# Sorting the first tokens of a scan-and-mixture kernel in two parts, and grouping the fp32 work of TensorE

## The chip, the cores and the metric

The kernel runs on one core of a Trainium2 chip. The metric is the device time of one execution in microseconds (us). Three runs of the kernel before gave 1382.56, 1383.54 and 1385.02 us (median 1383.54).

## What is computed

Three stages follow one another on N = 10112 tokens (2 sequences of 5056) of D = 256 values:

```
# stage A: a gated recurrence along each sequence
sig = 1.0 / (1.0 + np.exp(-f_logit))
f = lower_bound + (1.0 - lower_bound) * sig
h = f[:, t] * h + (1.0 - f[:, t]) * x[:, t]        # for t in range(S); y[:, t] = h
# layer 0: E = 8 experts of F = 1024, one expert for each token (cosine logits with tau)
xn = x / (np.linalg.norm(x, axis=-1, keepdims=True) + 1e-06)
logits = xn @ en.T / tau
expert_idx = np.argmax(logits, axis=1)
gate_w = softmax(logits)[arange(N), expert_idx]
out[mask] = gate_w[mask, None] * (np.maximum(x[mask] @ w1[e], 0.0) @ w2[e])   # per expert e
# layer 1: the same with other weights, and logits = x @ w_gate
```

## The kernel before

**Stage A, the scan.** Chunks of 512 tokens (CH = 4 tiles of P = 128; NCH = 20 chunks, the last of three tiles) are loaded as `xin` and `fin` (L737), transposed by TensorE (PE) into four PSUM banks (`a_front`, L1203: 16 transposes a chunk), and pass ScalarE's (ACT) tanh (L1049), GpSimd's (POOL) affine (L888) and VectorE's (DVE) product and scan (L371, L381). PE then transposes the result back (L1216) and computes the 8 logits of each token (L1222, `en_T`). ACT keeps the rows and their squares, and SP, the queue that issues most DMAs, stores the rows to `rows_a` in HBM (L745).

**A sort** puts the tokens of an expert together. A token's place ("slot") is found from counts: DVE finds the largest logit and a one-hot of the expert (`oh`, L413 to L419), PE counts with matmuls against ones and against an upper triangle (L1249, L1252), DVE turns the counts into slots (L432 to L464). Then a table "which row goes into which slot" is made. For each chunk of RC = 8 tiles, DVE and ACT build `tile_oh`, `lane_oh` and `vals` (`one_hots`, `scaled`), and PE accumulates 8 matmuls of 2 W columns (L1240). W is the number of 128-slot tiles that the table covers. Its two operands are read with a step of RC bf16 elements. DVE reads the table into `slot_row`. Each token's weight and number (`pair`) go to HBM as one store of 8 bytes a token beside the rows (`rows_a<-pair`, L813).

**The layers.** Slots are worked off in pairs of tiles (GW = 256 slots, one expert to a pair, NP = 47 pairs a layer, 94 in all). For each pair, SP reads the pair's expert from `expert` and loads 1 MB of `w1` and 1 MB of `w2` (`w1raw`, `w2raw`). ACT rounds them (`w1h`, `w2h`), and DVE takes the rest (`w1l`, `w2l`). POOL copies the pair's row numbers (`places`, L950) and gathers its rows by indirect DMA (`gather`, L966). PE transposes them (`turn_x`, L1290), and does `up` (L1306, 48 matmuls) and `down` (L1324, 48). In layer 0, ACT scales the result (`yb`), SP stores it to `rows_b`, and PE transposes it again (`turn_y`, L1344) and computes layer 1's logits (`y_logits`, L1335).

**What sets the order.** Each engine has its own written order. `step(i)` interleaves the work of pair i, of the pairs before it and of the next; each step has four points `tick(i, j)`, after the parts j = 0 to 3. A sort that runs beside the pairs is written as a generator on each engine, one `next` at each tick. Before, the first sort (`routing`, all TT = 79 tiles, W = 94) stands whole between scan and layer 0. The sort for layer 1 has two parts (`resort`): the first 64 tiles from step 34, for 16 whole pairs, and the rest from step 49, at the start of layer 1. Pair 0's weights are loaded at the end of the scan, as pair 0 always belongs to expert 0. POOL waits for `slot_row`, for the landing of the pair store and of the rows before it gathers.

Of the kernel before, what the change touches and what calls it, by code (L numbers as in the profile page):

```python
# [6 lines left out]
P = 128  # L7
# [45 lines left out]
def build(nc, x, f_logit, lower_bound, emb, tau, w1a, w2a, w_gate, w1b, w2b, out):  # L53
# [12 lines left out]
    G = 2  # L66
# [10 lines left out]
    UB = 2  # L77
    XA = 32
    GA = (N - (NP - XA) * GW - E * (GW - 1)) // GW
    TA, WA = G * XA, G * GA  # L80
# [12 lines left out]
    x_v = x.rearrange("b s d -> (b s) d").rearrange("(t p) d -> p t d", p=P)  # L93
    f_v = f_logit.rearrange("b s d -> (b s) d").rearrange("(t p) d -> p t d", p=P)

    ctx = ExitStack()
    with ctx:
# [7 lines left out]
        w1h = sb("w1h", [P, 2, WE], f32r)  # L105
        w1l = sb("w1l", [P, 2, WE], f32r)
        w2h = sb("w2h", [P, 2, WE], f32r)
        w2l = sb("w2l", [P, 2, WE], f32r)
# [25 lines left out]
        slot_tok = sb("slot_tok", [P, ST], fp32)  # L134
# [7 lines left out]
        hh = sb("hh", [P, JS, 512], f32r)  # L142
        hl = sb("hl", [P, JS, 512], f32r)
# [5 lines left out]
        sa = ExitStack()  # L149
        XS = UNROLL  # L150
        xin = sb("xin", [P, XS, CH * D], fp32, sa)
        fin = sb("fin", [P, XS, CH * D], fp32, sa)
        th = sb("th", [P, DC, CW], fp32, sa)
        fg = sb("fg", [P, DC, CW], fp32, sa)
        gx = sb("gx", [P, DC, CW], fp32, sa)
        sq = sb("sq", [P, 2, CH, D], bf16, sa)
        hT = sb("hT", [P, DC, 2, CW], fp32, sa)
        h_rows = sb("h_rows", [P, 2, CH * D], fp32, sa)
        sa.close()
# [3 lines left out]
        sr = ExitStack()  # L163
        lane_oh = sb("lane_oh", [P, RS, P, RC], bf16, sr)
        tile_oh = sb("tile_oh", [P, RS, ST, RC], bf16, sr)
        vals = sb("vals", [P, RS, 2 * ST, RC], bf16, sr)
        key = sb("key", [P, ST, E], fp32, sr)
        oh = sb("oh", [P, E, ST], bf16, sr)
        before = sb("before", [P, E, ST], fp32, sr)
        before2 = sb("before2", [P, E, ST], fp32, sr)  # L170
        small = sb("small", [P, 8, ST], fp32, sr)
        NORM_R, MAX_R, FIRST_R, SLOT_R, SUM_R, TMP_R, V0_R, OUT_R = range(8)
        ints = sb("ints", [P, 4, ST], i32, sr)
        e8 = sb("e8", [P, 8, E], fp32, sr)
        e8i = sb("e8i", [P, 2, E], i32, sr)
        cmp8 = sb("cmp8", [P, E, ST], fp32, sr)
        ex = sb("ex", [P, ST, E], fp32, sr)
        shifted = sb("shifted", [P, ST, E], fp32, sr)
        norm_e = sb("norm_e", [P, TT], fp32, sr)
        lane_rep = sb("lane_rep", [P, P, RC], bf16, sr)  # L180
        tile_rep = sb("tile_rep", [P, ST, RC], bf16, sr)
        where = sb("where", [P, 2, ST], bf16, sr)
        free = sb("free", [P, TA], bf16, sr)
        hole = sb("hole", [P, ST], fp32, sr)
        pair = sb("pair", [P, ST, 2], fp32, sr)
        sr.close()
# [3 lines left out]
        CUM_BANK, SUM_BANK = 2, 3  # L190
# [4 lines left out]
        pool_s = sem("pool_s")  # L195
        act_s = sem("act_s")
# [49 lines left out]
        PEEL_FIRST, PEEL_LAST = 3, 8  # L246
        SORT_FIRST, SORT_LAST = XA + 1, NP + GA - 2
# [3 lines left out]
        def part_of(r):  # L251

            if r == 0:
                return 0, TA, TA, WA, 0, GA
            return TA, ST, ST, ST - WA, GA, NP - GA

        def beside(part0, part1):

            def tick(i, j):
                if i.var is None and i.const * JS + j >= XA * JS + 2 * JS:  # L260
                    next(part0 if i.const < NP + 2 else part1, None)
            return tick

        FRONT = [18, 15]
# [26 lines left out]
        def run_pairs(eng, step):  # L291

            loop_layer[0] = 0
            run_steps(eng, 0, SORT_FIRST, step, PEEL_FIRST, 0, PAIR_UNROLL)
            loop_layer[0] = 1
            run_steps(eng, SORT_FIRST, LY * NP + 2, step, SORT_LAST - SORT_FIRST, PEEL_LAST, PAIR_UNROLL)
# [10 lines left out]
        CHUNK0 = [0, -(-TT // RC), -(-TT // RC) + -(-TA // RC), -(-TT // RC) + -(-TA // RC) + -(-ST // RC)]  # L307
# [3 lines left out]
        SPLIT_K = 3  # L311
        assert SPLIT_K + 1 < LOOP_K and NCH > LOOP_K + 4
# [5 lines left out]
        def _(dve):  # L318
# [32 lines left out]
            def split_w1_lo(i, c):  # L351

                cols = slice(c * F, (c + 1) * F)
                wait(dve, w1_hi, i.value(2, c + 1))
                v.tensor_tensor(w1l[:, par(i), cols], w1raw[:, par(i), cols],  # L355
                                w1h[:, par(i), cols].bitcast(fp32), ALU.subtract).then_inc(w1_lo, 1)

            def split_w2_lo(i, half):

                cols = slice(half * (WE // 2), (half + 1) * (WE // 2))  # L360
                wait(dve, w2_hi, i.value(2, half + 1))
                v.tensor_tensor(w2l[:, par(i), cols], w2raw[:, par(i), cols],  # L362
                                w2h[:, par(i), cols].bitcast(fp32), ALU.subtract).then_inc(w2_lo, 1)
# [31 lines left out]
            run_steps(dve, 0, edge_k, a_step, 6, 0)  # L395
            a_step(Index(edge_k), CH, edge_col)
            run_steps(dve, edge_k + 1, NCH - 1, a_step, max(LOOP_K - edge_k - 1, 0), 1)
# [1012 lines left out]
```

## Time and profile before

| | us |
|---|---|
| three runs, median | 1383.54 |
| the profiled execution, its own time | 1383.36 |
| its span, first to last instruction | 1381.6 |
| scan, to the last logits | 0 to 113 |
| first sort, to the first matmul of a pair | 113 to 169 |
| 94 pairs | 169 to 1380 |

PE is busy for 96% of the span, DVE 70%, ACT 60% and POOL 32%. Busy time says little of PE, whose matmuls overlap in the records. What counts is where PE waits, and how far the starts of its matmuls lie apart.

### The profile page before, as it was taken

The numbers are of one execution on the slowest core, as the hardware profiler recorded it, in microseconds if no ns is written. First come the engines' busy times: TensorE is split into PE (matmuls) and PEld (weight loads), VectorE is DVE, ScalarE is ACT, GpSimd is POOL, SyncE is SP. The second block draws the span as 40 slices with busy tenths as digits, with TensorE's granted clock in tenths as the row PEclk, the third lists the DMA queues.
The fourth block names the chain that finished last, engine by engine and source line by source line (L and its number), as shares of the span: only waits on it lengthen the run. The fifth ranks groups of instructions, "written<-read, shape, count | busy, mean of one in ns | idle before, by whom it ended". The sixth has DMA issues, their size and how long they took to land.

```text
span 1381.6 us, 31343 instructions
## 1 busy us (share of the span) xinstructions
PE 1329.6 (96%) x11005; PEld 1299.6 (94%) x11005; DVE 971.5 (70%) x1468; ACT 835.2 (60%) x1402; POOL 439.2 (32%) x458
## 2 busy tenths in 40 slices
PE   7994799999999999999999999999999999999996
PEld 6993399999999999999999999899999999999996
DVE  5878476666666666669876679777777777777773
ACT  4774166666666666666656566556666666666663
POOL 4663221121221211222111234323444444444431
PEclk9995599999999999999999999999999999999999
DMA  8983686666665656668856668546666666666650
GB/s 256 329 275 104 64 273 193 213 199 194 203 198 200 199 195 214 198 193 154 254 166 192 209 202 217 174 153 212 221 217 213 226 226 216 221 213 219 222 186 1
DMA packets 204662, 276.83 MB, mean 200 GB/s; under 512 B 33350, under 2 KB 171988, under 8 KB 204596
## 3 DMA queue, kind: packets, MB, share of 16 engines
q1 hardware_dynamic: 191060, 240.74, 56.7%
q0 software_dynamic: 13536, 35.21, 7.6%
q8 instruction: 41, 0.67, 0.2%
q14 instruction: 25, 0.20, 0.1%
HBM read 242.69 MB, written 35.18 MB: 201 GB/s over the span
## 4 chain that ended last, share of the span: by engine, by line
PE 91%; DVE 4%; issue 1%; ACT 1%; POOL 1%; DMA 1%; SPq 0%; ACTq 0%; DVEq 0%; POOLq 0%
PE bank L1306 39%; PE bank L1324 38%; PE bank L1240 4%; PE bank L1290 3%; PE bank L1335 2%; PE bank L1344 1%; PE bank L1203 1%; PE bank L1222 1%; PE bank L1216 1%; DVE hT L381 1%; DVE gx L371 1%; POOL fg L888 1%; ACT sq L1063 0%; DMA fin<-in_f_logit 0%; ACT th L1049 0%
## 5 line engine op out<-in xcount | busy, mean ns | idle before, releaser
L1306 PE MATMUL bank<-xs,w1h 128*128 128x256 f32 x3008 | 570.5, 288 | 1.5 <-DVE xs L656 1.5
L1119 ACT ACTIVATE hh<-bank 128x512 fp32r<-128x512 f32 x376 | 225.2, 599 | 413.6 <-PE bank L1306 413.6
L1306 PEld LDWEIGHTS bank<-xs,w1h 128*128 128x128 f32 x3008 | 461.5, 189 | 3.2 <-DVE xs L656 1.9
L667 DVE SCALAR_TENSOR_TENSOR hl<-bank,hh 128x512 fp32r<-128x512 f32 x376 | 259.9, 691 | 249.3 <-ACT hh L1119 246.9
L1324 PE MATMUL bank<-w2h,hl 128*128 128x256 f32 x1504 | 423.1, 281 | 0.0
L1324 PE MATMUL bank<-w2l,hh 128*128 128x256 f32 x1504 | 422.5, 281 | 0.0
L1324 PE MATMUL bank<-w2h,hh 128*128 128x256 f32 x1504 | 421.7, 280 | 0.0
L1306 PE MATMUL bank<-xs,w1l 128*128 128x256 f32 x1504 | 421.6, 280 | 0.0
L1306 PEld LDWEIGHTS bank<-xs,w1l 128*128 128x128 f32 x1504 | 283.7, 189 | 0.0
L1324 PEld LDWEIGHTS bank<-w2h,hh 128*128 128x128 f32 x1504 | 283.3, 188 | 0.0
L1324 PEld LDWEIGHTS bank<-w2l,hh 128*128 128x128 f32 x1504 | 283.1, 188 | 0.0
L1324 PEld LDWEIGHTS bank<-w2h,hl 128*128 128x128 f32 x1504 | 283.0, 188 | 0.0
L355 DVE TENSOR_TENSOR w1l<-w1raw,w1h 128x1024 fp32r<-128x1024 f32 x188 | 230.2, 1225 | 45.0 <-ACT w1h L1032 44.8
L362 DVE TENSOR_TENSOR w2l<-w2raw,w2h 128x1024 fp32r<-128x1024 f32 x188 | 230.4, 1226 | 43.1 <-ACT w2h L1040 42.2
L966 POOL DMA_INDIRECT xb<-rows_a,row_i x94 | 110.2, 1172 | 459.1 <-DVE meta L660 440.8
L976 POOL DMA_INDIRECT out_y<-yb,tok x94 | 125.8, 1338 | 313.0 <-DVE tok L675 282.9
L1032 ACT ACTIVATE w1h<-w1raw 128x1024 fp32r<-128x1024 f32 x188 | 197.6, 1052 | 7.1 <-DMA w1raw<-in_moe_w 7.1
L1040 ACT ACTIVATE w2h<-w2raw 128x1024 fp32r<-128x1024 f32 x188 | 197.6, 1052 | 0.8 <-DMA w2raw<-in_moe_w 0.8
L966 POOL DMA_INDIRECT xb<-rows_b,row_i x94 | 107.7, 1146 | 67.0 <-DVE meta L660 29.7
L1135 ACT ACTIVATE yb<-bank,meta 128x256 f32<-128x256 f32 x188 | 78.6, 470 | 11.4 <-PE bank L1324 4.5
L656 DVE TENSOR_TENSOR xs<-bank,xs 128x512 fp32r<-128x512 f32 x94 | 64.9, 690 | 11.5 <-ACT xs L1113 8.9
L1240 PE MATMUL bank<-vals,lane_oh 128*128 128x124 bf16 (+2 forms) x237 | 59.3, 415 | 10.7 <-DVE vals L511 10.5
(160 smaller groups left out, 1039.6 us busy)
## 6 DMA issues: line engine op xcount, KB each, us to landing
w1raw<-in_moe_w SPq DMA_DIRECT2D x94, 1024.0 KB
w2raw<-in_moe_w SPq DMA_DIRECT2D x94, 1024.0 KB, 5.6
rows_b<-yb SPq DMA_DIRECT2D x94, 128.0 KB, 2.3
xin<-in_x SPq DMA_DIRECT2D x19, 512.0 KB, 6.0
fin<-in_f_logit SPq DMA_DIRECT2D x19, 512.0 KB, 7.9
rows_a<-h_rows SPq DMA_DIRECT2D x19, 512.0 KB, 5.6
xb<-rows_a,row_i POOLq DMA_INDIRECT x94, 4.9
xb<-rows_b,row_i POOLq DMA_INDIRECT x94, 4.9
```

The lines of the kernel that those rows point to most:

```text
L355: v.tensor_tensor(w1l[:, par(i), cols], w1raw[:, par(i), cols], w1h[:, par(i), cols].bitcast(fp32), ALU.subtract).then_inc(w1_lo, 1)
L362: v.tensor_tensor(w2l[:, par(i), cols], w2raw[:, par(i), cols], w2h[:, par(i), cols].bitcast(fp32), ALU.subtract).then_inc(w2_lo, 1)
L667: v.scalar_tensor_tensor(hl[:, j, :], bank[j % UB][:, :], 0.0, hh[:, j, :].bitcast(fp32), ALU.max, ALU.subtract).then_inc(hid_lo, 1)
L966: pool.indirect_dma_start(xb[:, s, :], None, rows_of(i), bass.IndirectOffsetOnAxis(row_i[:, s:s + 1], 0)).then_inc(x_in[s], 16)
L976: pool.indirect_dma_start(out, bass.IndirectOffsetOnAxis(tok[:, s:s + 1], 0), yb[:, s, :], None, bounds_check=N - 1, oob_is_err=False).the ...
L1032: nc.scalar.activation(w1h[:, par(i), cols], w1raw[:, par(i), cols], ACT.Copy).then_inc(w1_hi, 1)
L1040: nc.scalar.activation(w2h[:, par(i), cols], w2raw[:, par(i), cols], ACT.Copy).then_inc(w2_hi, 1)
L1119: nc.scalar.activation(hh[:, j, :], bank[j % UB][:, :], ACT.Relu).then_inc(hid_hi, 1)
L1135: nc.scalar.activation(yb[:, s, :], bank[Y_BANK + par(i)][:, t * D:(t + 1) * D], ACT.Copy, scale=meta[:, bass.ds(in_layer(i).value(2 * G, ...
L1240: ins = mm(bank[b][:, 0:2 * W], lane_oh[:, g % RS, :, t], vals[:, g % RS, 0:2 * W, t], start=first and t == 0, stop=last and t == w - 1)
L1306: ins = mm(bank[j % UB][:, f * GW:(f + 1) * GW], w[:, p, o:o + P], xs[:, p, a, c * GW:(c + 1) * GW], start=k == 0, stop=k == 3 * DC - 1)
L1324: ins = mm(bank[Y_BANK + p][:, t * D:(t + 1) * D], a[:, j, f * GW + t * P:f * GW + (t + 1) * P], w[:, p, o:o + D], start=(j, t, f, k) == ( ...
```

## The change

1. The first sort has two parts. Part 0 takes the first K1 = 10 chunks (T1 = 40 tiles, 5120 tokens) and gives only whole pairs of one expert: P1 = 12 pairs, W = 24. It stands between scan and layer 0, where `routing` stood. Part 1 takes all 79 tiles for the other 35 pairs (W = 70); tokens already placed are masked. It runs at the ticks of steps 0 to 9 of layer 0, which are now written out instead of looped.
2. As pair 0's expert is no longer known beforehand, SP reads the experts of pairs 0 and 1 and loads both pairs' weights once part 0 has found the experts. The pair store of part 0 comes behind these four loads.
3. Both sorts of a layer are one generator (`sort(q)`, q = 0 to 3). Parts 1 and 3 count two experts at a time (four rounds between PE and DVE, in one bank), parts 0 and 2 four. Part 2 starts at step 35, part 3 at step 50.
4. In layer 0, `turn_y` (both tiles) and `y_logits` (both tiles, in a bank of their own, a step later) stand together behind `turn_x`. Before, they stood at four places of a step.
5. `xin` and `fin` are loaded so that a partition holds four consecutive tokens, 4 KB in one piece instead of four of 1 KB. The transposes put them back in order of time by writing every fourth column of the PSUM bank.
6. The number tables of POOL (`lane_rep`, `tile_rep`) are made ahead of the scan. `w1h` and the others are two buffers each, so that pair 0's lie apart from the scan's buffers.

```
-        SORT_FIRST, SORT_LAST = XA + 1, NP + GA - 2
+        PARTS = [(0, T1, T1, G * P1, 0, P1), (T1, TT, TT, ST - G * P1, P1, NP - P1),
+                 (0, TA, TA, G * PA, 0, PA), (TA, ST, ST, ST - G * PA, PA, NP - PA)]
+        FRONT = [20, 21, 22, 21]
+        OH_AT = [2, 2, 4, 2]
+        EXPERTS_AT_ONCE = [4, 2, 4, 2]
...
+            def tick(i):
+                if i.var is None and i.const >= NP + 3:
+                    next(parts[3], None)
+                elif i.var is None and i.const >= XA + 3:
+                    next(parts[2], None)
+                elif i.var is None and i.const < XA:
+                    next(parts[1], None)
...
 # SP
-                if i.var is None and i.const == NCH - 1:
-                    load_w1(Index(0))
-                    load_w2(Index(0))
+            def sort(q):
+                lo, hi = PARTS[q][0:2]
+                for _ in range(OH_AT[q] + 2 * len(groups(q)) + 6):
+                    yield
+                if q == 0:
+                    sp.wait_ge(dve_c, mark["experts", q])
+                    for i in (Index(0), Index(1)):
+                        read_expert(i)
+                        load_w1(i)
+                        load_w2(i)
+                        yield
+                sp.wait_ge(dve_c, mark["pair", q])
+                sp.dma_start((rows_av if q < 2 else rows_bv)[:, lo:hi, D:D + 2], pair[:, lo:hi, :]
+                             ).then_inc(pair_out, 16)
...
 # POOL, ahead of the first gather
-            pool.wait_ge(dve_c, mark["slots"])
+            pool.wait_ge(dve_c, mark["slots", 0])
             pool.wait_ge(pair_out, 16)
...
 # PE, a_front
+                        in_time = dst[:, 0:nt * P].rearrange("p (q j) -> p q j", j=nt)
                         for j in range(nt):
-                            ins = nc.tensor.transpose(dst[:, j * P:(j + 1) * P],
+                            ins = nc.tensor.transpose(in_time[:, :, j],
...
 # PE, the counting matmuls of a sort
+                for b, e, k, number in groups(q):
+                    if b == 0:
+                        pe.wait_ge(dve_c, mark["oh", q])
+                    else:
+                        pe.wait_ge(dve_c, mark["counted", q, b - 1])
+                    mm(sum_of(q, T), ones_b[:, :], oh[:, e:e + k, 0:T], start=True, stop=True)
+                    mm(cum_of(q, T), upto[:, :], oh[:, e:e + k, 0:T], start=True, stop=True).then_inc(pe_s, 1)
...
 # PE, step(i), behind turn_x
+                if here(old) and layer_of(old) == 0:
+                    y_logits(old)
                 if here(last2) and layer_of(last2) == 0:
-                    y_logits(last2, 1)
-                tick(i, 1)
+                    turn_y(last2)
+                tick(i)
```

SP's queue between the last stores of the scan (`rows_a<-h_rows`) and layer 0, before: pair 0's weights first, then the pair store, then pair 1's weights once the experts are read.

```order
L745 DMA rows_a<-h_rows 128x3x256 [waits rows_ok]
L759 DMA w1raw<-in_moe_w 128x2x1024
L767 DMA w2raw<-in_moe_w 128x8x256
L813 DMA rows_a<-pair 128x79x2 [waits dve_c]
L772 TENSOR_LOAD expert [waits dve_c]
```

The same place after:

```order
L719 DMA rows_a<-h_rows 128x3x256 [waits rows_ok]
L742 TENSOR_LOAD expert [waits dve_c]
L746 ISA
L729 DMA w1raw<-in_moe_w 128x2x1024
L746 ISA
L737 DMA w2raw<-in_moe_w 128x8x256
L742 TENSOR_LOAD expert
L746 ISA
L729 DMA w1raw<-in_moe_w 128x2x1024
L746 ISA
L737 DMA w2raw<-in_moe_w 128x8x256
L782 DMA rows_a<-pair 128x40x2 [waits dve_c]
```

No load stands ahead of the experts any more, and the pair store, of 40 tiles, has moved behind four loads of 1 MB.

PE in a step of layer 0 before, around `turn_x` (L1290), with one `y_logits` (L1335) behind it; the other `y_logits` and the two `turn_y` stand between other `up` and `down` groups.

```order
L1324 MATMUL bank<-w2l,hh 128x256
L1324 MATMUL bank<-w2h,hl 128x256
L1290 MATMUL bank<-ident,xb 128x128 x4
L1335 MATMUL bank<-wg_T,yT 128x8 x2
L1306 MATMUL bank<-xs,w1h 128x256 x2
L1306 MATMUL bank<-xs,w1l 128x256
```

The same place of a step in which part 1 of the first sort builds its table, after:

```order
L1269 MATMUL bank<-w2l,hh 128x256
L1269 MATMUL bank<-w2h,hl 128x256
L1235 MATMUL bank<-ident,xb 128x128 x4
L1282 MATMUL bank<-wg_T,yT 128x8 x4
L1292 MATMUL bank<-ident,yb 128x128 x4
L1214 MATMUL bank<-vals,lane_oh 128x140 x8
L1251 MATMUL bank<-xs,w1h 128x256 x2
L1251 MATMUL bank<-xs,w1l 128x256
```

All of a step's fp32 work is now one run, and behind it stand 8 table matmuls of 140 columns; there are ten such groups of up to 8 (79 matmuls) at the ticks of steps 5 to 8.

## Rows read from the trace of the kernel before

**Rows 1.** Windows by stage; the first row names the columns.
```profile
core 0: us, PE busy (x) PEld busy (x) DVE busy (x) ACT busy (x) POOL busy (x), PEclk, DMA share, GB/s
109.00:169.00 60.00, 33.20 (x105) 16.07 (x105) 41.34 (x82) 16.34 (x24) 16.54 (x12) 0.50 0.48 64
303.00:316.00 13.00, 13.00 (x114) 13.00 (x112) 8.42 (x13) 8.11 (x14) 2.43 (x3) 1.00 0.60 202
832.00:845.00 13.00, 12.70 (x107) 12.24 (x106) 12.06 (x21) 7.46 (x12) 5.64 (x5) 1.00 0.64 213
```

**Rows 2.** The chain in order of time, scan to layer 0: start, us, what.
```profile
116.38 3.10 DVE oh L419
...
123.03 0.18 DVE e8i L440
...
131.31 26.90 PE bank L1240 x79
...
158.52 0.27 DVE slot_row L485
...
163.71 3.11 DMA xb<-rows_a,row_i
...
169.04 5.02 PE bank L1306 x24
```

**Rows 3.** The chain in order of time, one step of layer 0.
```profile
303.19 0.44 PE bank L1290 x4
303.62 0.35 PE bank L1335 x4
303.97 1.51 PE bank L1306 x12
...
306.90 0.22 PE bank L1344 x2
307.12 1.40 PE bank L1306 x12
```

**Rows 4.** Timeline of DVE in the sort of 64 tiles beside layer 0.
```profile
615.71 0.68 DVE L535 TENSOR_REDUCE small<-logit 128x64 f32<-128x512 f32 x1
...
628.78 2.60 DVE L548 TENSOR_TENSOR oh<-key,small 128x512 bf16<-128x512 f32 x1
...
662.30 1.07 DVE L606 TENSOR_REDUCE small<-before 128x64 f32<-128x512 f32 x1
...
678.64 0.69 DVE L507 TENSOR_TENSOR lane_oh<-lane_rep,where 128x1024 bf16<-128x1024 bf16 x1
```

**Rows 5.** Timeline of SP: first and last of the four loads before layer 0.
```profile
165.96 0.39 SPq L759 DMA_DIRECT2D w1raw<-in_moe_w  x1
...
167.98 1.41 SPq L767 DMA_DIRECT2D w2raw<-in_moe_w  x1
```

**Rows 6.** DMA issues: KB each, median us to landing; third and fourth at 168 to 183.
```profile
rows_a<-pair SPq DMA_DIRECT2D x1, 79.0 KB, 15.3
rows_b<-pair SPq DMA_DIRECT2D x1, 64.0 KB, 14.8
...
w2raw<-in_moe_w SPq DMA_DIRECT2D x1, 1024.0 KB, 14.3
...
xb<-rows_a,row_i POOLq DMA_INDIRECT x5, 6.6
```

**Rows 7.** The chain, table matmuls beside layer 0 (64 columns) and layer 1 (124).
```profile
685.16 0.97 PE bank L1240 x8
...
908.90 1.84 PE bank L1240 x8
```

**Rows 8.** The chain in the scan: logits, and transposes at full and at half clock.
```profile
52.24 1.69 PE bank L1222 x16
...
68.57 1.80 PE bank L1203 x16
...
87.87 3.26 PE bank L1203 x16
```

More of the change, by code:

```diff
@@ L147, in build @@
         yT = sb("yT", [P, 2, D], fp32)
-        sa = ExitStack()
         XS = UNROLL
[L151 to L159, printed above, removed]
+        th = sb("th", [P, DC, CW], fp32)
@@ L161, in build @@
+        fg = sb("fg", [P, DC, CW], fp32)
+        gx = sb("gx", [P, DC, CW], fp32)
+        sq = sb("sq", [P, 2, CH, D], bf16)
         RC = 8
         RS = 4
[L163 to L169, printed above, removed]
@@ L180, in build @@
[L180 to L186, printed above, removed]
+        WM = ST - G * min(P1, PA)
+        lane_oh = sb("lane_oh", [P, RS, P, RC], bf16)
+        tile_oh = sb("tile_oh", [P, RS, WM, RC], bf16)
+        vals = sb("vals", [P, RS, 2 * WM, RC], bf16)
@@ new lines, in build @@
+        shifted = sb("shifted", [P, ST, E], fp32)
+        norm_e = sb("norm_e", [P, TT], fp32)
+        lane_rep = sb("lane_rep", [P, P, RC], bf16)
+        tile_rep = sb("tile_rep", [P, WM, RC], bf16)
+        where = sb("where", [P, 2, ST], bf16)
+        free = sb("free", [P, max(T1, TA)], bf16)
+        hole = sb("hole", [P, ST], fp32)
+        pair = sb("pair", [P, ST, 2], fp32)
+        scan_only = ExitStack()
+        xin = sb("xin", [P, XS, CH * D], fp32, scan_only)
+        fin = sb("fin", [P, XS, CH * D], fp32, scan_only)
@@ L1231, in _ @@
+            parts = [sort(q) for q in range(2 * LY)]
             run_steps(pe, 0, NCH, a_step, LOOP_K, 2)
             a_back(Index(NCH - 1), tiles_in(NCH - 1))
-            def chunk(g, w, W, b, first, last):
-                pe.wait_ge(lane_ok, g + 1)
-                pe.wait_ge(valp_ok, g + 1)
-                pe.wait_ge(valt_ok, g + 1)
-                for t in range(w):
-                    ins = mm(bank[b][:, 0:2 * W], lane_oh[:, g % RS, :, t], vals[:, g % RS, 0:2 * W, t],
-                             start=first and t == 0, stop=last and t == w - 1)
-                ins.then_inc(tab_ok, 1)
@@ L1358, in step @@
                     down(last, 2)
-                if here(last2) and layer_of(last2) == 0:
-                    turn_y(last2, 1)
-                tick(i, 0)
+                tick(i)
                 if here(i):
@@ L1373, in step @@
                     down(i, 0)
-                if here(last) and layer_of(last) == 0:
-                    turn_y(last, 0)
-                tick(i, 2)
+                tick(i)
                 if here(i):
```

664 lines of the change are left out of this document (308 added, 356 removed).

## The prediction

> **What bounds the kernel now.** I read the windows by stage first, then the chain that ended last. In layer 0 PE is busy for 13.00 of 13 us at full clock while DVE is busy for 8.42 [rows 1], and the chain of a step consists of PE groups that follow one another without a gap [rows 3]. So PE bounds both layers, and what DVE, ACT, POOL or a transfer does there costs nothing until it holds PE up. The windows give the margin too: where a sort runs beside the pairs, DVE is busy for 12.06 of 13 us [rows 1]. Between scan and layer 0 it is the other way round. PE is busy for 33.2 of 60 us at clock 0.50, the 1.2 GHz level [rows 1], and the chain goes through DVE's counting, 79 table matmuls (26.90), `slot_row`, the gather and the first `up` at 169.04 [rows 2]. The sort starts at S = 113.0, some 3.4 us ahead of `oh` at 116.38, so the lead-in is 56.0 us long. In the scan itself the chain goes through PE and the engines behind it, not through the loads: transposes 1.80 and logits 1.69 stand in it [rows 8].
>
> All changes are set against the profiled execution: span 1381.6, its own time 1383.36, 1.8 more; the median of the runs is 1383.54, 0.2 above that.
>
> **Start of the scan.** `xin` and `fin` in pieces of 4 KB land a little earlier, but only the first chunk is waited for: −0.3 (−0.6 to 0). The transposes into every fourth PSUM column I cost at nothing, and keep their price as a rival. POOL's number tables go where POOL was idle.
>
> **Lead-in, from S.** The first part sorts 40 tiles, 320 numbers a partition. DVE's wide operations shrink from 640 numbers: `oh` took 3.10 [rows 2], and 2.60 for 512 [rows 4], some 0.5 per 128 numbers, so 1.8. The lines of 512 numbers at 0.68 and 1.07 [rows 4] become about 0.5 and 0.7. Maximum to `oh` is then about 3.8, the norm 0.6, two counting rounds with PE 2.4, nine operations on 8 experts such as `e8i` at 0.18 [rows 2] 1.85, and the experts of the pairs 0.85: experts at S + 9.5. The slots take DVE another 9 or so, and five chunks of one-hots at 1.05 each (`lane_oh` 0.69 [rows 4] and a third of the other) 5.3. PE's 40 table matmuls of 48 columns hide behind these: 26.90/79 for 188 columns is 1.8 ns a column [rows 2], so 40 × 48 × 1.8 ns = 3.5. `slot_row` is ready at S + 24.2, against 45.5 before (158.52 [rows 2]).
>
> But POOL waits for the pair store too, and this is where the queue matters. SP issues four loads of 1 MB once the experts are there, then the pair store. Before, such four went from 165.96, the last issued at 167.98 and landed 14.3 later [rows 5, 6], so 16.3 from first to last, gathers among them; without gathers I take 14.5. The pair store is behind them in the queue. It took 15.3 for 79 tiles and 14.8 for 64 [rows 6]. In proportion to the tiles 40 would take 7.7, by the line through the two 14.0. The issue and the first descriptors pass beside the loads, so I take 6.5 behind them. That gives S + 9.5 + 14.5 + 6.5 = S + 30.5, 6 us after the slots: **the end of the pair store takes the place of the slots**. Then row numbers (0.9), two gathers beside what is left of the traffic at 6.6 (the median [rows 6]; 3.11 alone [rows 2]) and transposes, rounding and start of `up` 2.2: first `up` at S + 40.2. Against S + 56.0 that is −15.9. Bounds: −21.5, slots at S + 24.2 and nothing else late; −12, a store that takes nearer 14.
>
> **Part 1 on PE in layer 0.** Of the 79 table matmuls none is saved. They are 140 columns wide now and stand between PE groups that never wait. Eight took 0.97 at 64 columns and 1.84 at 124 [rows 7], 0.0145 a column; at 140 that is 1.84 + 16 × 0.0145 = 2.07. Then 79/8 × 2.07 = 20.4. The eight counting matmuls add 0.7 and a wait at the first chunk 0.3: +21.4, less 0.1 as the last group is one matmul short: +21.3 (20 to 24). This is the term that decides: what was beside nothing, 26.90 in the lead-in, costs 20 in a place where PE is full.
>
> **DVE in steps 0 to 3.** The key, `oh` and exp work of part 1 on 640 numbers is about 4.6 in one step, on top of 8.8 of split work: 13.3 against a step of 11 to 13 without `turn_y`. PE stalls +1.2 (0 to 4). Steps 6 and 7 have four chunks of one-hots each, for DVE some 4 × 1.1 on top of 8.42 [rows 1], in a step that four groups of table matmuls stretch to 21; that fits. The slots stand at the ticks of step 8 and POOL reads them at step 9, a step of some 13 us later: no wait.
>
> **fp32 work together.** Before, a step has `turn_x` 0.44, two logits matmuls 0.35 (four records, two to a matmul), and `up` behind them 1.51 where it is 1.40 elsewhere: 0.11 for going back. `turn_y` 0.22 stands apart, with `up` behind it at 1.40 [rows 3]. With the second logits and `turn_y` that comes to 0.44 + 2 × 0.35 + 2 × 0.11 + 2 × 0.22 = 1.80. After, the logits are eight records in a row. In the scan 16 in a row take 1.69 [rows 8], 0.106 each against 0.35/4 = 0.088, so eight take 0.80 to 0.85: 0.44 + 0.80 + 0.44 + 0.11 = 1.79. If two groups of 0.35 stay what they are, it is 1.69. The ends for 47 steps are thus −5 and, with 0.85, +2; I take −1.5. It is a small gain, since `turn_y` had no delay behind it to give up.
>
> **Second sort.** Part 3 counts in four rounds, a step apart, and starts a step later: −0.2 (−0.5 to +0.5), both within what DVE had free.
>
> **Sum.** −0.3 − 15.9 + 21.3 + 1.2 − 1.5 − 0.2 = +4.6. Span 1386.2, with 1.8 around it 1388.0, +0.3%.
>
> **Rivals.** *A, the pair store is not in the way.* Its descriptors might be carried beside the four loads, or the loads be so far down that it lands before the slots. The first `up` then comes by the slots: S + 24.2 + 0.9 + 3.1 to 6.6 + 2.2, near S + 34.5 with part of the contention. That is −21.5 instead of −15.9, in all 1382.4; with the −5 end of the fp32 work 1379. So it ends at not slower, or faster. For it: 79 tiles took 15.3 alone, 64 took 14.8 beside layer traffic, so traffic hardly slowed it [rows 6]. Against: that traffic was not four loads ahead in its own queue. It decides from where the store lands before S + 25, 15.5 us after the experts. 0.25.
>
> *B, the strided transposes are slow.* The transposes now write fp32 columns 16 bytes apart. No row shows such a write. If each took as long as at half clock, 3.26 in place of 1.80 for 16 [rows 8], the 20 chunks would cost 20 × 1.46 = 29 less what slack PE has in a chunk, some 0.2 to 0.4: +25, in all 1412. It decides from about 0.4 us a chunk, beyond PE's slack. Against it: a matmul's output is written once a column, 1.8 ns apart at most when strided operands are read [rows 7], and ACT and POOL read the bank packed as before. The Trainium skill, Advanced Engine Details and Errata, section PSUM Cachelines, says that any non-contiguous access pattern significantly slows down matmuls, with lines of two fp32 values; no run here has yet shown it. By that rule the time would be near this rival's, without it the forecast's. 0.11.
>
> *C, DVE or gathers too late in steps 0 to 5.* The pair store of 39 tiles in step 4 and DVE's 4.6 of extra work fall where weights for the next pairs must be split. Two or three steps that end on DVE at 13.3 to 15 instead of PE at 11 to 13 cost +5, in all 1392. The store of 64 tiles cost PE nothing beside layer 0, where PE stayed full. 0.07.
>
> *D, the change does not do what it says.* The slots of part 1 come too late for pair 12, so the pairs wait for the sort after all, for half a step or more: 1395. A step between writing and reading speaks against it. 0.03.
>
> **How the numbers follow.** The forecast has 0.54: 1388.0, by itself 1384 to 1393 from the ends of the lead-in (−21.5 to −12) and of DVE and fp32. A's times reach from 1379 to 1384. The range is 1380 to 1393: it leaves out B, D and the lowest part of A. A measurement of this kernel tells 0.2%, 2.8 us, from no change: faster is below 1380.8, slower above 1386.3. Faster takes half of A and little of the forecast, 0.14; within 0.2% the rest of A and a third of the forecast, 0.28; slower two thirds of the forecast with B, C and D, 0.58.
>
> **What would show it.** Lead-in: the gather's end in the chain comes from `pair_out` and not from `slot_row`; the pair store lands some 6 us after the slots; first `up` 40 us after S. If the chain goes through `slot_row`, A is right. Part 1: nine groups of table matmuls near 2.07 and one of 7 in the chain of steps 5 to 8; steps 6 and 7, with four each, near 21 us. DVE: an idle stretch of PE in step 0 or 1 that ends on `w1l`, `w2l` or `h`. fp32: in layer 0's chain `turn_x` 0.44, logits x8 0.80, `turn_y` 0.44 and `up` behind them 1.51; logits of 0.70 would show the end of −5. Scan: 1.80 a group of 16 transposes, with S still near 113; at 3 or above, B. I would be wrong at the root if table matmuls of 140 columns between `up` groups took nearer 1 us for eight, or if first `up` came later than S + 44.

## The result, and the profile after

The changed kernel took 1389.4 us (median of 6 runs, 1386.44 to 1395.21) against 1383.9 for the kernel before (6 runs): ratio 1.0045, 95% interval 1.0034 to 1.0057. In a later series of 10 runs it took 1386.6 against 1384.1: 1.0018, interval 1.0008 to 1.0028. So it is slower, by 0.2 to 0.5% (2.5 us in one series, 5.5 in the other); the forecast was 1388.0, +0.3%.

The profiled execution happened to be the slowest of the first series (1395.21, span 1393.5). The profile of the second series (1386.23, span 1384.5) is near the median and stands for the changed kernel from here on, called the second profile. The lines of code are numbered anew: `turn_x` is L1235, `up` L1251, `down` L1269, `y_logits` L1282, `turn_y` L1292, the table matmuls L1214, the counting matmuls L1201 and L1202.

The difference to the kernel before, stretch by stretch, from the starts of `turn_x` of single pairs in both traces (us):

| stretch | before | after, second profile | difference |
|---|---|---|---|
| start to `turn_x` of pair 0 | 165.30 | 152.41 | −12.9 |
| to pair 2 | 20.30 | 23.75 | +3.5 |
| pairs 2 to 6 | 51.95 | 50.31 | −1.6 |
| pairs 6 to 9 (tables of part 1) | 39.29 | 59.37 | +20.1 |
| pairs 9 to 34, plain steps of layer 0 | 327.32 | 323.95 | −3.4 |
| pairs 34 to 62 (second sort, change of layer) | 380.62 | 380.77 | +0.2 |
| pairs 62 to 92, plain steps of layer 1 | 353.60 | 350.90 | −2.7 |
| rest | 43.2 | 43.0 | −0.2 |

Chain of the second profile from scan to layer 0 (start, us, what), beside [rows 2]:

```profile
113.28 0.18 DVE logit L434
...
123.25 0.18 DVE expert L535
...
126.83 18.17 DMA rows_a<-pair
145.13 0.31 POOL row_i L912 x2
...
146.03 6.24 DMA xb<-rows_a,row_i
152.41 1.10 PE bank L1235 x4
```

S, the end of the copy of the last logits, is 113.5. The experts stand at S + 9.9, the pair store lands at S + 31.5, and the first `up` begins at 154.90, S + 41.4. The slots were ready long before: `slot_row` ends at 137.3, S + 23.8. Nothing of the table matmuls is in the chain; the store is.

One plain step of layer 0 in its chain, beside [rows 3], and table matmuls of 140 columns, beside [rows 7]:

```profile
389.68 0.44 PE bank L1235 x4
390.12 0.79 PE bank L1282 x8
390.91 0.49 PE bank L1292 x4
391.40 1.41 PE bank L1251 x12
...
255.24 2.07 PE bank L1214 x8
```

The windows of the second profile, beside [rows 1]: the lead-in is shorter and still at the 1.2 GHz level, the layer is as full as before.

```profile
core 0: us, PE busy (x) PEld busy (x) DVE busy (x) ACT busy (x) POOL busy (x), PEclk, DMA share, GB/s
108.00:155.00 47.00, 10.85 (x70) 8.77 (x70) 27.49 (x78) 10.34 (x27) 7.49 (x10) 0.51 0.66 166
385.00:398.00 13.00, 13.00 (x114) 13.00 (x113) 8.46 (x12) 8.11 (x12) 2.16 (x3) 1.00 0.61 205
```

What was open: how much of the result is noise of the scan, whether the store is really what the gather waits for, what the stall ahead of pair 2 is, why plain steps of **both** layers became shorter though only layer 0's fp32 work was moved, and whether the table matmuls must cost 20 us.

### The profile page after: what moved, and what is told of

Read it like the earlier page. It is cut to its first block, busy times and chain, and to the rows that moved or that the text cites. A ratio compares the mean times of both kernels' runs of the same rounds, so it can differ in the third digit from the quotient of the medians.

```text
span 1393.5 us, 31206 instructions
## 1 busy us (share of the span) xinstructions
PE 1326.5 (95%) x11057; PEld 1304.2 (94%) x11057; DVE 984.9 (71%) x1497; ACT 826.0 (59%) x1361; POOL 419.3 (30%) x461
## 4 chain that ended last, share of the span: by engine, by line
PE 91%; DVE 4%; DMA 2%; issue 1%; POOL 1%; ACT 1%; DVEq 0%; POOLq 0%; ACTq 0%
PE bank L1269 38%; PE bank L1251 38%; PE bank L1214 4%; PE bank L1235 3%; PE bank L1282 3%; PE bank L1164 2%; PE bank L1183 2%; PE bank L1292 2%; DMA rows_a<-pair 1%; PE bank L1177 1%; DVE hT L426 1%; DVE gx L416 1%; POOL fg L860 0%; DMA xb<-rows_a,row_i 0%; DVE oh L487 0%
## 5 line engine op out<-in xcount | busy, mean ns | idle before, releaser
L1251 PE MATMUL bank<-xs,w1h 128*128 128x256 f32 x3008 | 559.7, 285 | 1.4 <-DVE xs L618 1.4
L1251 PEld LDWEIGHTS bank<-xs,w1h 128*128 128x128 f32 x3008 | 464.6, 190 | 4.4 <-DVE xs L618 1.8
L1269 PE MATMUL bank<-w2h,hl 128*128 128x256 f32 x1504 | 422.4, 281 | 0.0
L1269 PE MATMUL bank<-w2h,hh 128*128 128x256 f32 x1504 | 421.9, 281 | 0.0
L1251 PE MATMUL bank<-xs,w1l 128*128 128x256 f32 x1504 | 421.8, 280 | 0.0
L1269 PE MATMUL bank<-w2l,hh 128*128 128x256 f32 x1504 | 421.6, 280 | 0.0
L1251 PEld LDWEIGHTS bank<-xs,w1l 128*128 128x128 f32 x1504 | 285.0, 189 | 0.0
L1269 PEld LDWEIGHTS bank<-w2h,hh 128*128 128x128 f32 x1504 | 283.9, 189 | 0.0
L1269 PEld LDWEIGHTS bank<-w2h,hl 128*128 128x128 f32 x1504 | 283.7, 189 | 0.0
L1269 PEld LDWEIGHTS bank<-w2l,hh 128*128 128x128 f32 x1504 | 283.7, 189 | 0.0
L928 POOL DMA_INDIRECT xb<-rows_a,row_i x94 | 96.5, 1027 | 488.3 <-DVE meta L622 457.7
L938 POOL DMA_INDIRECT out_y<-yb,tok x94 | 123.0, 1308 | 313.1 <-DVE tok L640 283.1
L928 POOL DMA_INDIRECT xb<-rows_b,row_i x94 | 101.3, 1078 | 69.5 <-DVE meta L622 42.2
L1235 PE MATMUL bank<-ident,xb 128*128 128x128 f32 x376 | 56.8, 274 | 16.9 <-DMA xb<-rows_a,row_i 16.9
```

The costliest lines, as they stand in the source:

```text
L928: pool.indirect_dma_start(xb[:, s, :], None, rows_of(i), bass.IndirectOffsetOnAxis(row_i[:, s:s + 1], 0)).then_inc(x_in[s], 16)
L938: pool.indirect_dma_start(out, bass.IndirectOffsetOnAxis(tok[:, s:s + 1], 0), yb[:, s, :], None, bounds_check=N - 1, oob_is_err=False).the ...
L1235: ins = nc.tensor.transpose(bank[X_BANK][:, o:o + P], xb[:, s, c * P:(c + 1) * P], ident[:, :])
L1251: ins = mm(bank[j % UB][:, f * GW:(f + 1) * GW], w[p][:, o:o + P], xs[:, p, a, c * GW:(c + 1) * GW], start=k == 0, stop=k == 3 * DC - 1)
L1269: ins = mm(bank[Y_BANK + p][:, t * D:(t + 1) * D], a[:, j, f * GW + t * P:f * GW + (t + 1) * P], w[p][:, o:o + D], start=(j, t, f, k) == ( ...
```

## The experiments

Ratios are to the kernel before, in the same series.

**The changed kernel again.**

> The changed kernel once more. Its profiled execution took 1395.21 us, 5.8 above its median 1389.4, and its scan ended 6.6 us later than that of the kernel before. Theory 1 (the late scan belongs to that execution, the changed loads cost little): here the last logits are kept within 2 us of 113, the profiled time is 1387 to 1391, and the steps of the layers are the same as before to 0.02 us. Theory 2 (the changed loads and transposes cost it): the scan ends at 117 or later again.

1386.59 us, ratio 1.0018 (1.0008 to 1.0028), 10 runs. The scan ends at 113.3, as theory 1 has it. In the first profile it ended at 119.4, and the chain shows where that came from:

```profile
20.60 3.21 PE bank L1183 x16
23.81 3.51 PE bank L1164 x16
```

In the second profile the same two groups stand at 20.35 with 1.69 and at 22.04 with 1.80. In every profile PE's first groups take twice the time of later ones (3.66 for 16 transposes at 8.44 before, 3.58 at 9.96 after), up to 19 or 20 us; in this one it goes on to 28. These are the durations that stretches at the half clock have in [rows 8], though the windows print a granted clock of 1.00 for that stretch. Of the nine profiles with the changed start four have it (the first, and those of the old loads, of the store first and of the changed kernel with the tables in rows); their last logits are copied at 117.0 to 119.4. The five others with that start (112.2 to 114.3) and the five with the start as before (110.2 to 112.8) don't. What differs at the start is one operation. DVE's `emb_q` took 0.40 us before and takes 2.66 now, since POOL makes `lane_rep` and `tile_rep` at that moment, from the chain and the timeline of POOL in the second profile:

```profile
6.43 2.66 DVE emb_q L383
...
5.94 1.94 POOL L879 IOTA lane_rep<- 128x1024 bf16 x1
7.83 1.10 POOL L879 IOTA tile_rep<- 128x560 bf16 x1
```

PE's first transposes begin at 9.96 instead of 8.44. That the later start makes the long slow stretch more frequent fits all 14 profiles, but four in nine against none in five can be chance, and it was not tried by itself.

The traces differ in one more place. In four of them (the first profile and, of the experiments below, the old loads, the store first and `vals` in rows) the granted clock falls to half once, for some 3 us, among the table matmuls of part 1. In the first three of these PE does not wait there, and pairs 6 to 9 take 60.8 to 60.9 us, against 59.4 in the second profile. Single executions of the changed kernel so differ by several us for reasons that the change does not fix, and the stretches of the table above are the surer ground.

**fp32 work apart again.**

```
 # PE, step(i), of the changed kernel; ACT and DVE follow
+                if here(last2) and layer_of(last2) == 0:
+                    turn_y(last2, 1)                      # behind down(last, 2)
...
-                if here(old) and layer_of(old) == 0:
-                    y_logits(old)
                 if here(last2) and layer_of(last2) == 0:
-                    turn_y(last2)
+                    y_logits(last2, 1)
```

> The changed kernel with the fp32 work of layer 0 at four places of a step, as before the change. A plain step of layer 0 took 13.09 us before and 12.96 after; one of layer 1, which has no such work, 11.79 and 11.70. Theory 1 (grouping gives 0.04 a step, the rest has another cause that acts in both layers): layer 0 steps of 13.00 to 13.01, layer 1 steps still 11.70, the kernel 2 us slower than the changed one. Theory 2 (grouping gives the whole 0.13): layer 0 steps of 13.09, 6 us slower.

1387.56 us, ratio 1.0028 (1.0014 to 1.0041). Pairs 9 to 34 take 325.60 us, 13.02 a step, against 323.95, 12.96. So grouping gives 0.066 a step, 3.1 us in 47 steps. The medians of the two kernels (1387.56 and 1386.59) are too close to show so much; it rests on the steps, which repeat to 0.01 us from trace to trace. The 0.066 is half of the 0.13 by which the steps of layer 0 became shorter. Steps of layer 1 are 11.70 in both. Theory 1 holds. In the chain of this kernel the delay behind logits is there again, and none behind `turn_y`:

```profile
404.23 0.35 PE bank L1281 x4
404.57 1.48 PE bank L1252 x12
...
407.48 0.22 PE bank L1290 x2
407.69 1.37 PE bank L1252 x12
```

**The weights placed as after.**

```
-        w1h = sb("w1h", [P, 2, WE], f32r)
+        w1h = [sb("w1h0", [P, WE], f32r)]
...
         pair = sb("pair", [P, ST, 2], fp32, sr)
+        for n, t in (("w1h", w1h), ("w1l", w1l), ("w2h", w2h), ("w2l", w2l)):
+            t.append(sb(n + "1", [P, WE], f32r, sr))
+        hh = sb("hh", [P, JS, 512], f32r, sr)
+        hl = sb("hl", [P, JS, 512], f32r, sr)
```

> The kernel before with one edit: the rounded weights are two buffers each, and the second ones and hh and hl stand at the end of SBUF, as after the change. Theory 1 (matmuls of up and down take 113 ns instead of 117 to 120 for some positions of their operands in SBUF): steps of layer 1 about 11.70 instead of 11.79, of layer 0 about 13.00 instead of 13.09, the kernel 6 to 8 us faster than before, near 1376. Theory 2 (the gain of 0.09 a step comes from the rewritten order of the steps): steps as before, time as before.

1388.56 us, ratio 1.0034 (1.0024 to 1.0044): slower. Steps of layer 0 take 13.16 instead of 13.09, of layer 1 11.81 instead of 11.79. Neither theory: places alone do move every step, but this placement, which is not the changed kernel's to the byte, moves them the other way. The next experiment on this is the last one.

**Loads and transposes of the scan as before.**

```
-                        in_time = dst[:, 0:nt * P].rearrange("p (q j) -> p q j", j=nt)
-                            ins = nc.tensor.transpose(in_time[:, :, j],
+                            ins = nc.tensor.transpose(dst[:, j * P:(j + 1) * P],
```

> The changed kernel with xin and fin loaded in pieces of 1 KB and transposes that write 128 columns in a row, as before the change. Theory 1 (both edits of the scan are about free): 16 transposes at full clock 1.80 us in either, end of the scan within 1 us of that of the changed kernel in the same clock, total within 2 us. Theory 2 (writes into every fourth PSUM column are slow, rival B of the prediction): the changed kernel would be slower than this one, by 5 us or more.

1389.8 us (6 runs), ratio 1.0038 (1.0021 to 1.0055), not faster than the changed kernel. At full clock 16 transposes take 1.80 us in this kernel, in the changed one and in [rows 8], and its profile has the long slow stretch at 20 to 28 us too (3.21 and 3.51). So neither the 4 KB pieces nor the writes into every fourth PSUM column have a price that can be seen, and they are not what makes the scan late. The Trainium skill, Advanced Engine Details and Errata, section PSUM Cachelines, has any non-contiguous access slow matmuls significantly; for fp32 transposes written 16 bytes apart the two traces do not show it.

**The pair store first.**

```
+                sp.wait_ge(dve_c, mark["pair", q])
+                sp.dma_start((rows_av if q < 2 else rows_bv)[:, lo:hi, D:D + 2], pair[:, lo:hi, :]
+                             ).then_inc(pair_out, 16)
                 if q == 0:
-                    sp.wait_ge(dve_c, mark["experts", q])
                     for i in (Index(0), Index(1)):
```

(The same two statements behind the loop are gone.)

> The changed kernel with the pair store of part 0 ahead of the four weight loads in SP's queue instead of behind them. In the second run of the changed kernel the slots were read at S + 24, the pair store landed at S + 31.7 and the first up began at S + 41.6. Theory 1 (the store waits behind the loads in its queue and holds the gather): it lands before the slots, the chain goes through slot_row, first up near S + 32 to S + 34, the kernel 8 to 9 us faster than the changed one, near 1379. Theory 2 (8-byte packets are slow wherever they stand, and weights are needed as much): the landing moves to S + 25 at best, the loads come 4.3 us later and the first up waits for w1l, gain under 4 us.

1382.43 us, ratio 0.9993 (0.9976 to 1.001). S is 117.5 in its profile, after the slow stretch. The store lands 9.8 us after its issue at 128.73, at S + 21.0, ahead of the slots (S + 23.8). The first `up` begins at 152.13, S + 34.6, and the gather now starts behind the slots:

```profile
139.98 0.93 PE bank L1213 x8
...
141.61 0.32 POOL row_i L911 x2
...
143.63 6.34 DMA xb<-rows_a,row_i
...
152.13 2.94 PE bank L1250 x12
```

That is 6.8 us earlier against S than in the changed kernel, and up to pair 2 nothing of it comes back (21.07 us from first `up` to the third `turn_x`, against 21.26). So the mechanism is theory 1. The gain in time, though, is not the 8 to 9 us expected: against the kernel before, the medians are 0.1 us lower here and 2.5 or 5.5 higher for the changed kernel, a gain of 2.6 to 5.6 with runs that spread from 1376.5 to 1387.4. The two variable stretches named above (slow start, clock among the tables) are both in this profile; how much of the shortfall they are in the other runs was not traced. The windows show why the place in the queue matters: in the second profile of the changed kernel the loads move 373 GB/s with the store behind them, and from 138 on it is alone, with a DMA share of 2.00 for 8 GB/s (the share adds up the times of packets, and can exceed 1). With the store first it has that phase at 130, while DVE still counts. Two rows of the changed kernel, then one of this one:

```profile
130.00:132.00 2.00, 0.00 (x0) 0.00 (x0) 1.83 (x9) 0.45 (x1) 0.00 (x0) 0.50 1.11 373
138.00:140.00 2.00, 0.00 (x0) 0.00 (x0) 2.00 (x3) 1.29 (x2) 0.00 (x0) 0.50 2.00 8
```

```profile
130.00:132.00 2.00, 0.00 (x0) 0.00 (x0) 1.90 (x8) 0.00 (x0) 0.00 (x0) 0.50 0.76 13
```

**Part 1 two ticks later.**

```
-        FRONT = [20, 21, 22, 21]
-        OH_AT = [2, 2, 4, 2]
+        FRONT = [20, 23, 22, 21]
+        OH_AT = [2, 4, 4, 2]
...
-                if q == 2:
+                if q in (1, 2):
                     yield
```

> The changed kernel with part 1 of the first sort two ticks later from its key on, so that PE's first counting matmul (which waited 4.5 us for DVE's oh at step 1, and 2.4 for the masked oh) stands two ticks, half a step, later. Theory 1 (PE's stall of steps 0 and 1 is that wait): from first up to the third turn_x 17 to 18.5 us instead of 21.3, the kernel 3 us faster than the changed one. Theory 2 (DVE is simply overloaded there, and another of its products would be waited for, w1l or hl): still 20 to 21 us, no change in time.

1382.85 us, ratio 1.0007 (0.9996 to 1.0018), 0.3 us above the kernel before where the changed kernel is 2.5 above: a gain of 2.2, 3 expected. The expectation named a wrong wait: the 4.5 us for `oh` belong to part 0, in the lead-in. Part 1's is the wait for the masked `oh` (L490). From first `up` to the third `turn_x` it takes 16.7 us instead of 21.3, so theory 1 holds. Of these 4.6 us only 2.4 were idle. The windows of the changed kernel and then of this one show the rest, PEclk is the third number from the end:

```profile
164.00:168.00 4.00, 2.38 (x21) 2.19 (x19) 3.97 (x6) 1.55 (x2) 1.82 (x1) 1.00 0.81 262
168.00:172.00 4.00, 3.20 (x22) 3.21 (x23) 3.61 (x7) 1.28 (x2) 1.88 (x3) 0.79 0.28 71
172.00:176.00 4.00, 4.00 (x29) 4.00 (x29) 2.39 (x5) 1.31 (x3) 0.00 (x0) 0.79 0.78 258
```

```profile
164.00:168.00 4.00, 4.00 (x36) 4.00 (x36) 3.96 (x7) 1.67 (x3) 2.52 (x2) 1.00 0.87 276
168.00:172.00 4.00, 4.00 (x37) 4.00 (x36) 3.96 (x5) 2.77 (x4) 1.40 (x2) 1.00 0.62 192
172.00:176.00 4.00, 3.78 (x34) 3.55 (x33) 3.86 (x9) 2.95 (x6) 0.73 (x1) 1.00 0.74 203
```

Behind the wait the granted clock is 0.79 for 8 us: part of them ran at 1.2 GHz again, right after the clock had come back. That does not follow each time. In the kernel with the fp32 work apart PE waits 2.3 us at the same place and in the one with `vals` in rows (below) 2.1, and in both the clock stays at full speed. From first `up` to the third `turn_x` they take 19.7 us, against 16.6 before and 21.3 here. One group behind the wait, in the second profile and in the kernel with the fp32 work apart:

```profile
168.80 0.24 PE bank L1201
...
170.68 2.56 PE bank L1269 x12
```

```profile
169.72 0.24 PE bank L1202
...
171.49 1.41 PE bank L1270 x12
```

So of the 4.6 us some 2.4 are the wait and 1.6 the clock. The last 0.6 is not gained at all: counting matmuls now stand two ticks later, and pairs 2 to 6 take 50.95 us instead of 50.31.

**The tables' moving operand in a row.** First only `vals`, with its writes then strided, in the changed kernel and in the kernel before:

```
-        vals = sb("vals", [P, RS, 2 * WM, RC], bf16)
+        vals = sb("vals", [P, RS, RC, 2 * WM], bf16)
...
-                v.tensor_tensor(vals[:, g % RS, 0:W, 0:w], tile_oh[:, g % RS, 0:W, 0:w],
+                v.tensor_tensor(vals[:, g % RS, 0:w, 0:W].rearrange("p r w -> p w r"), tile_oh[:, g % RS, 0:W, 0:w],
```

> The changed kernel with the table matmuls' moving operand vals kept so that PE reads its 140 (48, 64, 124) columns in a row instead of with a step of 8; DVE and ACT write it with the step instead. Theory 1 (the step sets 1.8 ns a column): eight matmuls of 140 columns take about 1.0 us or less instead of 2.07, as then the weights bound them, part 1 costs PE near 10 us instead of 20.6, part 3 of the second sort near 12 instead of 22, the kernel 18 to 22 us faster than the changed one, near 1367. Theory 2 (the weights lane_oh, read with a step too, or the width itself sets the time): 2.07 stays, and DVE's and ACT's writes get longer: same or slower.

> The kernel before with the same packed vals and nothing else. Theory 1: the 79 table matmuls of the first sort (26.9 us in the chain) fall to where DVE's one-hots bound them, 10 chunks of some 1.5 us, slot_row 8 to 10 us earlier; the second sort gives 10 us; the kernel near 1364, so that with cheap table matmuls the split in two parts would still bring nothing. Theory 2: 1384 or more.

1379.86 us, ratio 0.9988 (0.9973 to 1.0003), and for the kernel before 1411.19, ratio 1.0205 (1.0188 to 1.0222). Neither came near its expectation (1367 and 1364). Where PE does not wait inside a group, eight table matmuls of 140 columns now take about 0.5 us from the first's start to the next group's, instead of 1.84 (2.07 in the chain). But DVE's write costs 2.81 for 560 elements, where it was 0.44, and 3.47 for 752:

```profile
244.40 2.81 DVE L451 TENSOR_TENSOR vals<-tile_oh,tileno 128x560 bf16<-128x560 bf16 x1
```

```profile
130.44 3.47 DVE L511 TENSOR_TENSOR vals<-tile_oh,tileno 128x752 bf16<-128x752 bf16 x1
```

Beside the layers part of that hides, but not all: in the steps of part 1 PE waits 7.5 us for DVE's `vals`. In the lead-in of the kernel before nothing does: its slots are 17.9 us later against the same logits, and its second sort costs another 12.8. My sum for that kernel had priced the matmuls and not the writes, and was wrong by 47 us.

Then `tile_oh` and `vals` both in rows, so that all reads and writes of PE, ACT and DVE go in a row and only DVE's second operand repeats:

```
-                v.tensor_tensor(vals[:, g % RS, 0:W, 0:w], tile_oh[:, g % RS, 0:W, 0:w],
-                                tileno[:, t0:t0 + w].unsqueeze(1).to_broadcast([P, W, w]),
+                v.tensor_tensor(vals[:, g % RS, 0:w, 0:W], tile_oh[:, g % RS, 0:w, 0:W],
+                                tileno[:, t0:t0 + w].unsqueeze(2).to_broadcast([P, w, W]),
...
-                        ins = mm(table_of(q, T, W), lane_oh[:, g % RS, :, t], vals[:, g % RS, 0:2 * W, t],
+                        ins = mm(table_of(q, T, W), lane_oh[:, g % RS, :, t], vals[:, g % RS, t, 0:2 * W],
```

> The changed kernel with tile_oh and vals both kept as 8 rows of W columns, so that PE and ACT read them in a row and DVE and ACT write them in a row; DVE's second operand is then the one that repeats from column to column. With only vals packed, eight table matmuls took 0.92 us instead of 2.07, but DVE's write of vals 3.5 in the kernel before (2 x 188 columns) and DVE was busy for 28 of 21 us in steps 7 and 8. Theory 1 (DVE writes in a row stay cheap, some 0.6 us for 560 elements instead of 0.39): 0.92 stays, steps 7 and 8 take 16.7 us instead of 21.1, part 3's steps 14.5 to 15.5 instead of 17.2, the kernel 18 to 24 us faster than the changed one. Theory 2 (the operand that repeats costs DVE as much as the write did): gain of 6 us as with only vals packed, or less.

> The kernel before with the same tile_oh and vals. Theory 1: in its first sort the chain goes through DVE's one-hots, 10 chunks of some 2.3 us instead of 26.9 us of table matmuls, slot_row 3 to 6 us earlier, the second sort 10 to 12 us cheaper: 15 us faster than before, near 1368. Set against the changed kernel with the same edit it tells what the two parts are worth when a table matmul is cheap: there part 1 costs PE 9 us instead of 21 and the lead-in still gives 13 to 15, so that kernel should be 5 us faster or more. Theory 2: the repeated operand is slow, no gain or a loss.

1363.45 us, ratio 0.9864 (0.9847 to 0.988); the kernel before with it 1370.6, ratio 0.9925 (0.9908 to 0.9941). DVE's two lines take 0.72 or 0.73 instead of 0.44, the matmuls 0.57 for eight. From the timeline of DVE and the chain of the changed kernel with this edit:

```profile
250.38 0.72 DVE L451 TENSOR_TENSOR vals<-tile_oh,tileno 128x560 bf16<-128x560 bf16 x1
...
251.66 0.57 PE bank L1214 x8
255.12 0.57 PE bank L1214 x8
```

Pairs 6 to 9 take 45.36 us instead of 59.37. With cheap tables the changed kernel is 7 us (0.5%) ahead of the kernel before with the same edit, where it was 2.5 to 5.5 behind. That is not all due to the split in two parts. From the traces of the two kernels: the lead-in is 12.1 us shorter (53.6 to 41.5), from first `up` to the third `turn_x` it takes 4.9 more (there PE waited 3.3 us for the masked `oh`, and the clock fell), pairs 2 to 6 take 1.1 less and pairs 6 to 9 6.1 more. So the split gives 2 us at most; 1.5 of them are work on `y` that only comes later (see below). Another 5.0 come from pairs 34 to 62, the second sort, where only the kernel before with this edit waits for DVE:

```profile
PE bank L1240 <- DVE vals L511: 6.4, 9, 1.0
```

(PE waited 6.4 us in all, nine times, at most 1.0.) The gain from grouping is not to be seen between these two: the places of buffers have moved again, and plain steps take 13.07 and 11.81 us against 13.09 and 11.79.

The Trainium skill, Advanced Engine Details and Errata, section SBUF Cachelines, has an operand that touches another 16-byte line at each access pay for it. The traces agree: with a step of 16 bytes a column takes 2.07/8/140 = 1.8 ns, and the same 1.8 ns at a granted clock of 0.50 [rows 1, 2]. In a row eight matmuls of 140 columns take 0.57, so a column costs 0.51 ns at most. It may cost less, as the width no longer matters: in the kernel with all three edits, groups of eight take 0.46 to 0.53 us to the next group's start at 64, at 124 and at 140 columns.

**All three edits.**

> The changed kernel with three edits: tile_oh and vals in rows, the pair store ahead of the four loads, part 1 two ticks later. If the gains are of separate places they add up: 7 us from the store, 4 from the counting matmuls' wait, 18 to 24 from the tables, near 1355. If DVE, which carries all three, is the next bound, the sum falls short by 5 us or more, with idle time of PE in steps 1 to 9.

1355.02 us, ratio 0.9821 (0.98 to 0.9843), faster than both kernels. The total is the one expected, 1355. The first `up` begins at S + 35.5, pair 2's `turn_x` 16.9 us later, and pairs 6 to 9 take 44.1 (two of the ten groups of table matmuls now stand behind pair 9). DVE stays just behind the pace: PE waits 0.1 us in steps 1 to 9.

**32 bytes.**

```
+        sb("pad", [P, 8], fp32)
         w1raw = sb("w1raw", [P, 2, WE], fp32)
```

> The kernel before with 32 bytes of unused SBUF behind w2l, so that all later buffers, xs, hh and hl among them, move by 32 bytes against w1h to w2l. Theory 1 (where the operands lie in SBUF sets 113 or 117 to 120 ns a matmul, as the kernel with placed weights suggests, 11.82 us a step of layer 1 instead of 11.79): steps of layer 1 move by 0.03 us or more. Theory 2 (it was the instructions, not the places): 11.79 stays.

1367.33 us in its one run, against a median of 1381.39 for the kernel before in that series. Steps of layer 1 take 11.58 instead of 11.79, of layer 0 12.96 instead of 13.09, and that accounts for it: 47 × 0.21 + 47 × 0.13 = 16 us, and the span is 16.0 shorter. It is one execution, but its plain steps agree among themselves to 0.02 us, as those of the kernel before do. Half a step of layer 1 in the chain of the kernel before, then the same in this one; two of the four groups are down, from 1.42 and 1.41 to 1.38 and 1.36, and so are two of the other four:

```profile
1032.52 1.43 PE bank L1306 x12
1033.95 1.42 PE bank L1324 x12
1035.37 1.41 PE bank L1306 x12
1036.78 1.42 PE bank L1324 x12
```

```profile
1068.77 1.42 PE bank L1307 x12
1070.19 1.38 PE bank L1325 x12
1071.56 1.36 PE bank L1307 x12
1072.92 1.42 PE bank L1325 x12
```

No instruction has changed but the addresses of buffers. So where they lie in SBUF sets whether a matmul follows the one ahead of it after 113 to 115 or after 117 to 119 ns (groups of 1.36 to 1.38 or of 1.40 to 1.43, over twelve). Which buffer matters was not tried.

## Why the prediction was right, term by term

The direction and the size were right: +4.6 forecast for the span, +2.9 in the second profile. But only three terms behind the sum held (bound, lead-in, part 1). The errors of the others nearly cancelled, and that the total came so near is luck.

- **What bounds the kernel**: held. The lead-in became shorter, and PE, full in the layers, had to take part 1.
- **Lead-in**, −15.9 forecast: −14.6 measured (56.0 to 41.4). The step that carried it held in detail: experts at S + 9.5 (9.9), slots at S + 24.2 (23.8), store landed at S + 30.5 (31.5), first `up` at S + 40.2 (41.4). That the store takes the place of the slots is shown by putting it first. The first `up` then came at S + 34.6, where rival A had put it (34.5) for a store out of the way. That number is better than its working, whose terms add up to 30.4 to 33.9: from the slots to the start of the gather it took 2.3 us and not 0.9. A was wrong in its condition: in that queue the store is in the way.
- **Part 1 on PE**, +21.3: eight at 140 columns took 2.07, as worked out from 64 and 124 columns. Pairs 6 to 9 are 20.1 longer, 20.5 with their plain steps taken at 12.96.
- **DVE in the first steps**, +1.2 (0 to 4): +4.7 in the second profile, beyond its own range. The wait was 2.4 us, within the bounds. What I left out is that PE's clock can fall again behind it. Where it did not, in two of the other traces, the term is +3.1, within the range; the clock adds 1.6.
- **fp32 work**, −1.5 (−5 to +2): −3.1, by the experiment. The mechanism was mis-sized. I gave the delay of 0.11 to any fp32 group ahead of `up`. In the traces it stands behind logits (1.51 against 1.40) and not behind `turn_y`, so with `turn_y` last both delays go, not one. Part of that returns as longer logits (0.79) and `turn_y` (0.49).
- **Start of the scan**, −0.3, and POOL's tables at nothing: wrong. The last logits come 0.5 us later in the second profile, and 6.6 in the first. The tables went where POOL was idle, but DVE was not: `emb_q` took 2.66 instead of 0.40.
- **Not in the sum at all**: 0.07 of the 0.13 us a step in layer 0, and the whole 0.09 in layer 1, together −7.5 us. They are not the grouping. The edit of the tables is a further sign that it is places: in that kernel nothing is changed in a plain step, but `tile_rep` is smaller and what lies behind it in SBUF moves; its steps are 13.07 and 11.81 again. That places can do this is shown by 32 bytes. That it was the places in the changed kernel follows from these, and was not tried by itself; which rule they follow stays open.
- **Second sort**, −0.2: nearer to +1.7. Pairs 34 to 62 are 0.2 longer, although shorter steps should have made them 3 us shorter; 1.5 of the difference are logits of three tiles and the `turn_y` of one pair that now come later (pairs 2 to 6 have as many fewer, and are 1.6 shorter), and the rest are waits such as 1.1 us of PE behind the change of layer.

Rival B (strided transposes) fell with the loads put back. The argument against it took its spacing from the wrong matmuls: the transposes write a column every 1.80/16/128 = 0.88 ns, not every 1.8. C's mechanism, DVE too late in the first steps, was there at 3.1 to 4.7 of its 5 us, with the wait at a counting matmul and not at weights. D did not occur: pair 12 does not wait.

So the sum came out within 2 us because errors cancelled: the stall (3.5 more than forecast), the second sort (1.9), the lead-in (1.3) and the scan (0.8) against the places and the fp32 work (9.1 less).

## What to carry to other kernels

Moving work from a phase in which an engine waits to one in which it is full gains only if the work is first made cheap: here the table matmuls were priced by the stride of their operand, and with rows instead the changed kernel is 7 us ahead of its rival and no longer behind, but only 2 of them or less come from the split, and 5 from the second sort. A small store that a gather waits for belongs ahead of the large loads in its queue: here that brought the gather 6.8 us forward. And before steps of two kernels are compared to 1%, see whether buffers have moved: here 32 bytes of SBUF were worth more than the whole change.

## What the hardware showed that I had not expected

- Shifting buffers by 32 bytes changed a step with 96 matmuls of `up` and `down` from 11.79 to 11.58 us.
- Table matmuls whose operand is read with a step of 16 bytes take 1.8 ns a column at either level of the clock; in a row, eight of them take 0.46 to 0.53 us whether they have 64 or 140 columns.
- Behind a wait of 2.4 us the clock fell back to half, and the stretch took 4.7 us more than before; behind waits of 2.1 and 2.3 at the same place it did not, and the stretch took 3.1 more.
- A bf16 write of DVE with a large step took 2.81 us for 560 elements, 0.44 with the packed operands of before, and 0.72 with one operand that repeats.
- A store in packets of 8 bytes keeps the DMA engines busy at 8 GB/s (share 2.00), where loads move 373 (share 1.11).
